# A fused Fourier transform and two expert layers on one core: three sequence passes and two means move in among the first items of the first tile

## The reference

```python
def _attn_ref(x):                        # x (2, 3008, 256)
    X = np.fft.fft(x, axis=1)
    X = np.fft.fft(X, axis=2)
    return X.real
def _moe_ref(x, w_gate, w_val, w_out, rms_g):      # d_ff 1536
    rms = np.sqrt(np.mean(x * x, axis=-1, keepdims=True) + 1e-06)
    xn = x / rms * rms_g
    g = xn @ w_gate
    silu = g * (1.0 / (1.0 + np.exp(-g)))
    return (silu * (xn @ w_val)) @ w_out
def _moe2_ref(x, w_in, w_out):                     # d_ff 2048
    h = x @ w_in
    return (h * np.cos(h)) @ w_out
```

## Time and profile before

| | |
|---|---|
| median of three runs | 978.87 us |
| the profiled execution's own time | 978.91 us |
| its span in the trace | 977.0 us |
| PE busy | 971.1 us (99%) |
| DVE, ACT, POOL busy | 742.1, 638.3, 350.6 us |
| granted PE clock | 0.999 |

### The profile page before, as it was taken

One profiled execution on the slowest core, in us unless ns is written; L12 is line 12 of the kernel. 1 busy time (PEld: TensorE's weight loads), 2 busy tenths in 40 slices (PEclk: granted clock), 3 DMA queues, 4 the chain that ended last, 5 costly groups with the idle time before them and its releaser, 6 DMA issues.

```text
span 977.0 us, 13033 instructions
## 1 busy us (share of the span) xinstructions
PE 971.1 (99%) x4530; PEld 808.7 (83%) x4530; DVE 742.1 (76%) x1029; ACT 638.3 (65%) x806; POOL 350.6 (36%) x291
## 2 busy tenths in 40 slices
PE   9999999999999999999999999999999999999998
PEld 8988888888888888888888888888888888888886
DVE  7888987678876768876768877767887667887665
ACT  5687787764378765368775358775348776447777
POOL 0477783047720027740007750006661004770000
PEclk9999999999999999999999999999999999999999
DMA  9888010001010001010001000001010000000001
GB/s 356 232 223 218 1 39 16 1 2 41 1 42 1 1 1 42 1 42 0 0 0 42 0 32 11 0 0 42 0 32 0 0 0 20 22 0 0 0 0 42
DMA packets 13794, 36.80 MB, mean 38 GB/s; under 512 B 2586, under 2 KB 6522, under 8 KB 13370
## 3 DMA queue, kind: packets, MB, share of 16 engines
q1 hardware_dynamic: 11690, 31.63, 9.3%
q0 software_dynamic: 2064, 4.72, 2.6%
HBM read 22.35 MB, written 9.26 MB: 32 GB/s over the span
## 4 chain that ended last, share of the span: by engine, by line
PE 98%; DVE 1%; DMA 0%; ACT 0%; issue 0%; DVEq 0%
PE ps L554 31%; PE ps L555 31%; PE ps L556 31%; PE ps L500 2%; PE ps L518 1%; PE ps L484 1%; PE ps L516 1%; DMA front<-x 0%; DVE plus L1028 0%; PE ps L540 0%; ACT g_sb L683 0%; DVE work L1036 0%; PE ps L481 0%; PE ps L480 0%; DVE work L1037 0%
## 5 line engine op out<-in xcount | busy, mean ns | idle before, releaser
L556 PE MATMUL ps<-h_hi,wo_lo 128*128 128x502 f32 x672 | 261.5, 389 | 0.0
L554 PE MATMUL ps<-h_hi,wo_hi 128*128 128x502 f32 x672 | 261.4, 389 | 0.0
L555 PE MATMUL ps<-h_lo,wo_hi 128*128 128x502 f32 x672 | 261.0, 388 | 0.0
L1127 POOL TENSOR_TENSOR h_lo<-work,h_hi 128x502 fp32r<-128x502 f32 x92 | 102.2, 1119 | 373.8 <-ACT h_hi L807 370.2
L792 ACT ACTIVATE h_hi<-work 128x502 fp32r<-128x502 f32 x132 | 82.2, 626 | 172.0 <-POOL work L1216 172.0
L1114 DVE SCALAR_TENSOR_TENSOR work<-work,ps 128x1004 f32<-128x1004 f32 (+1 forms) x109 | 117.2, 1075 | 95.3 <-ACT work L893 94.6
L1100 DVE SCALAR_TENSOR_TENSOR work<-work,ps 128x1004 f32<-128x1004 f32 (+1 forms) x109 | 116.5, 1074 | 48.4 <-ACT work L879 48.4
L554 PE MATMUL ps<-x_hi,win_hi 128*128 128x502 f32 x384 | 150.0, 391 | 0.0
L555 PE MATMUL ps<-x_lo,win_hi 128*128 128x502 f32 x384 | 149.4, 389 | 0.0
L556 PE MATMUL ps<-x_hi,win_lo 128*128 128x502 f32 x384 | 149.1, 388 | 0.0
L554 PEld LDWEIGHTS ps<-h_hi,wo_hi 128*128 128x128 f32 x672 | 126.2, 188 | 26.8 <-DVE h_lo L1021 0.6
(11 more groups left out here) (92 smaller groups left out, 1271.8 us busy)
## 6 DMA issues: line engine op xcount, KB each, us to landing
out<-y_sb SPq DMA_DIRECT2D x10, 502.0 KB, 3.2
front<-x SPq DMA_DIRECT2D x4, 768.0 KB, 9.0
w_lo<-w_f POOLq DMA_DIRECT2D x6, 512.0 KB, 7.0
uv_t<-uv_dram SPq DMA_DIRECT2D x6, 502.0 KB, 3.6
front<-x SPq DMA_DIRECT2D x4, 512.0 KB, 9.0
wo_raw<-wo SPq DMA_DIRECT2D x1, 2048.0 KB, 9.3
win_raw<-win SPq DMA_DIRECT2D x1, 2048.0 KB, 10.4
raw_b<-w1b SPq DMA_DIRECT2D x3, 512.0 KB, 12.6
```

The source lines that it names most:

```text
L554: nc.tensor.matmul(acc, w_hi, v_hi, start=start, stop=False)
L555: nc.tensor.matmul(acc, w_hi, v_lo, start=False, stop=False)
L556: return nc.tensor.matmul(acc, w_lo, v_hi, start=False, stop=stop)
L1127: nc.gpsimd.tensor_tensor(dst, src, hi.bitcast(F32), ALU.subtract).then_inc(s, 1)
```

## The change

What the edits do:

- `sequence(31)` is taken from before the first item and put into item 1; `sequence(32)` and `(33)` each move one place later. `rms(6)`, done at step 33 before, is done together with `rms(7)` inside item (2, 1), between the sum and the difference, in banks 6 and 7.
- On ACT, `uv_copy(15)` goes from before the first Silu to behind it; `mean_copy(6)` and `(7)` come behind `hi1(0)`.
- `pq` becomes four buffers, three of them behind `uv0` and one 2 KB behind `plus[0]`, so that `plus[0]` has bytes of its own.
- Two more weight slots, `w1_late0` and `w1_late1`, lie in the part of `wo1_hi` and `wo1_lo` that chunk 2 of wo1 fills later. Mixings no longer wait for `w1_lo_done`; chunks 4 and 5 are split on ACT in items 0 and 1 instead of 1 and 2; `split_wo1(2)`, in item 4, now waits for `w1_lo_done[4]` and `[5]`.
- Scalings and mixings are at other steps (the last two mixings at 25 and 33, not 31 and 32), and three small DVE instructions on the scale vectors come behind the copies of the transform's last groups.

```diff
@@
+        w1_late = [sb(f"w1_late{i}", [2, 512], o + 8192) for i, o in enumerate((o_o1h, o_o1l))]
+        def w1_slot(n):
+            return w1_f[:, n, :, :] if n < SLOTS else w1_late[n - SLOTS][:, :, :]
@@
-        pq = sb("pq", [4, DIM], o_pq)
+        pq = [sb(f"pq{i}", [DIM], o_h + UVB + 1024 * i if i < 3 else o_pq + 2048) for i in range(4)]
@@
-        RMS_AT = [8, 9, 15, 20, 24, 28, 33]
-        MEAN_COPY_AT = [2, 3, 7, 9, 11, 13, 14]
+        RMS_AT = [8, 9, 15, 20, 24, 28]
+        MEAN_COPY_AT = [2, 3, 7, 9, 11, 13]
@@
-            return 3 if q < len(RMS_AT) else 6 if q < MEANS - 1 else bank_pair(1)
+            return 3 if q < len(RMS_AT) else q if q < MEANS - 1 else bank_pair(1)
@@
-        MIX_AT = [3, 5, 8, 9, 16, 18, 20, 22, 24, 25, 31, 32]
+        MIX_AT = [3, 5, 7, 9, 11, 16, 18, 20, 22, 24, 25, 33]
...
-        W1_SPLIT_LATE, WO1_SPLIT_LATE = {1: 4, 2: 5}, {3: 1, 4: 2}
+        W1_SPLIT_LATE, WO1_SPLIT_LATE = {0: 4, 1: 5}, {3: 1, 4: 2}
@@ PE
-                if q == RMS_LATE[0]:
+                if q in RMS_LATE[:2]:
                     pe.wait_ge(uv_main, LAST - 2)
@@
-            sequence(LAST - 3)
@@
                 if first:
                     up1_sum(t, 1, 0)
-                    sequence(LAST - 2)
+                    sequence(LAST - 3)
                     up1_dif(t, 1, 0)
                     up1_sum(t, 1, 1)
-                    sequence(LAST - 1)
+                    sequence(LAST - 2)
                     up1_dif(t, 1, 1)
                     up1_sum(t, 2, 0)
-                    rms(RMS_LATE[0])
+                    sequence(LAST - 1)
                     up1_dif(t, 2, 0)
@@
-                    up1(t, i, halves=(1,))
+                    up1_sum(t, i, 1)
+                    if first and i == 2:
+                        rms(RMS_LATE[0])
+                        rms(RMS_LATE[1])
+                    up1_dif(t, i, 1)
@@ ACT
+                if n == WO1_CHUNKS - 1:
+                    act.wait_ge(w1_lo_done[SLOTS], 16)
+                    act.wait_ge(w1_lo_done[SLOTS + 1], 16)
@@
-            for p in range(LAST // 2 - 1):
+            for p in range(LAST // 2 - 2):
...
+            split_step(LAST // 2 - 2)
@@
+                    if first and i == 1:
+                        mean_copy(RMS_LATE[0])
+                        mean_copy(RMS_LATE[1])
                     act.wait_ge(g_ready, C1 * t + i + 1)
...
                     if first and i == 0:
+                        uv_copy(LAST // 2 - 2)
                         uv_copy(LAST // 2 - 1)
-                        mean_copy(RMS_LATE[0])
...
                     if first and i in W1_SPLIT_LATE:
                         split_w1(W1_SPLIT_LATE[i])
@@ DVE
-                if k // 2 >= SLOTS:
-                    dve.wait_ge(w1_lo_done[k // 2 - SLOTS], 16)
```

More of the change, by code:

```diff
@@ L111, in build @@
         wo1_raw = sb("wo1_raw", [C1 * DIM], o_i2h)
+        w1_late = [sb(f"w1_late{i}", [2, 512], o + 8192) for i, o in enumerate((o_o1h, o_o1l))]
+        assert WO1B == 3 * 4096 and 2 * FF1 == (SLOTS + 2) * 512
+        def w1_slot(n):
+            return w1_f[:, n, :, :] if n < SLOTS else w1_late[n - SLOTS][:, :, :]
         win2_hi, win2_lo = sb("win2_hi", [2 * FF2], o_i2h, F32R), sb("win2_lo", [2 * FF2], o_i2l, F32R)
@@ L154, in build @@
         o_pq = o_h + 4 * TA
-        pq = sb("pq", [4, DIM], o_pq)
+        pq = [sb(f"pq{i}", [DIM], o_h + UVB + 1024 * i if i < 3 else o_pq + 2048) for i in range(4)]
+        assert UVB + 3 * 1024 <= 4 * TA and 4 * N <= 2048
         zeros = sb("zeros", [P], o_pq)
@@ L237, in part_end, with parts_ending @@
             return b * STEPS + k.stop - 1
-        RMS_AT = [8, 9, 15, 20, 24, 28, 33]
-        MEAN_COPY_AT = [2, 3, 7, 9, 11, 13, 14]
+        def parts_ending(p):
+            return [q for q in range(MEANS) if part_end(q) // 2 == p]
+        RMS_AT = [8, 9, 15, 20, 24, 28]
+        MEAN_COPY_AT = [2, 3, 7, 9, 11, 13]
         RMS_LATE = range(len(RMS_AT), MEANS)
@@ L243, in build @@
         RECIP_LATE = {7: 1, 9: 2}
-        assert len(RMS_LATE) == 2
+        assert len(RMS_LATE) == 3 and not parts_ending(LAST // 2 - 2)
         def rms_bank(q):
-            return 3 if q < len(RMS_AT) else 6 if q < MEANS - 1 else bank_pair(1)
+            return 3 if q < len(RMS_AT) else q if q < MEANS - 1 else bank_pair(1)
         def rounds(q):
@@ L256, in quarters @@
             return min(4, PART_ROWS[q][1].stop - PART_ROWS[q][1].start) * QUARTER
-        def parts_ending(p):
-            return [q for q in range(MEANS) if part_end(q) // 2 == p]
         def means_copied(p):
@@ L515, in sequence @@
                 bank = 4 + G % 4
-                nc.tensor.matmul(ps[:, bank, 0:N2], pq[0:2 * H, slot(G), 0:P],
+                nc.tensor.matmul(ps[:, bank, 0:N2], pq[slot(G)][0:2 * H, 0:P],
                                  seq2[0:2 * H, k1, :], start=True, stop=True)
-                nc.tensor.matmul(ps[:, bank, N2:2 * N2], pq[0:2 * H, slot(G), P:DIM],
+                nc.tensor.matmul(ps[:, bank, N2:2 * N2], pq[slot(G)][0:2 * H, P:DIM],
                                  seq2[0:2 * H, k1, :], start=True, stop=True).then_inc(uv_done, 1)
@@ L650, in tile @@
                     if first and i == LAST_MEAN_AT:
-                        rms(RMS_LATE[1])
+                        rms(RMS_LATE[2])
                 down(t, C1 - 2)
@@ L741, in split_w1 @@
                 act.wait_ge(mixed, 2 * n + 2)
-                nc.scalar.activation(w1_hi[:, :, c], w1_f[:, n % SLOTS, :, :], ACT.Copy).then_inc(w1_hi_done, 1)
+                nc.scalar.activation(w1_hi[:, :, c], w1_slot(n), ACT.Copy).then_inc(w1_hi_done, 1)
                 if n >= W1_EARLY:
@@ L838, in tile @@
                     if first and i == LAST_MEAN_AT:
-                        mean_copy(RMS_LATE[1])
+                        mean_copy(RMS_LATE[2])
                     if first and i in W1_SPLIT_LATE:
@@ L1135, in w1_add @@
                     pool.wait_ge(w1_neg_late, n - W1_EARLY + 1)
-                pool.dma_start(w1_lo[:, :, c], w1_f[:, n % SLOTS, :, :], accum_op=ALU.add
+                pool.dma_start(w1_lo[:, :, c], w1_slot(n), accum_op=ALU.add
                                ).then_inc(w1_lo_done[n], 16)
```

18 lines of the change are left out of this document (9 added, 9 removed).

## The result

The changed kernel takes 980.47 us (median of 20 runs, 980.10 to 985.43), the kernel before 979.04 us (20 runs, 978.70 to 980.71). The forecast was 979.9 us. The profiled execution took 980.46 us with a span of 978.7 us, at a granted clock of 1.00, so it stands for the median, and the two spans differ by 1.7 us.

The account below looks back on a forecast made before the run. PE was taken to bound the first tile, with 0.7 us margin on the ACT chain before `down(0)`. Terms -0.12 + 0.88 + 0.3 gave +1.06 on 978.91: 979.97, median 979.9; 8-in-10 range 978.2 to 981.9.

Parts of the forecast that it names:

- The sum: Whole kernel: -0.12 + 0.88 + 0.3 = +1.06 us on the profiled 978.91, giving 979.97, or 979.9 for the median.
- the forecast's own range: Whole kernel: 979.2 to 980.8 us, for a late first `down` plus 0 to 0.9 of DMA waits; chance 0.56.
- main term: At `down(0)`: PE starts at 67.0 instead of 66.14, held by ACT's longer chain through `hi1(0)`; +0.88 us.
- Reading: First tile after 65.30: PE idles 0.06 us of 64.40, so earlier changes return one for one unless a new wait opens.
- Part 1: End of the transform: three small DVE instructions leave the place before the copy; between 0 and -0.28 us, taken as -0.12.
- Part 2: First item: its `pq` is no longer behind a mixing, so PE starts at 54.77, 0.87 us sooner.
- Part 3: PE before `down(0)`: with `sequence(31)` and `rms(6)` moved in, it could start at 65.7, 0.45 us sooner.
- Part 4: ACT before `hi1(0)`: uv copies and a split delay it to 65.2, `down(0)` to 67.0, +0.88; `down(1)` costs nothing.
- Part 5: DMA landings around `down(4)`: chunk 5 between 80.8 and 86.3, wo1's chunk 1 possibly late; 0.3 us for both.
- Rival A: At `down(0)`: ACT's new chain ends before PE needs it, so the gain arrives; -0.6, 978.3 us; chance 0.14.
- Rival B: At `down(4)`: ACT or PE waits for a DMA landing in full queues; up to 2.2 more, 981.8 us; chance 0.23.
- The rule of the Trainium skill: At `down(4)`: queues take turns, so an accumulating DMA beside one load takes about twice its time; no stall past the forecast.

Follow-up runs that it names:

- e1: Changed kernel with chunks 4 and 5 of the first weights split in items 1 and 2, not 0 and 1; 980.88 us, ratio 1.0019.
- e9: Changed kernel with the three small DVE instructions back in front of the transform's last copies; 980.63 us, ratio 1.0017.
- e2: Changed kernel with ACT's eight splits of the second input weights in items 7 to 10 instead of 6 to 9; 980.11 us, ratio 1.0016.
- f1: Changed kernel with the earlier kernel's weights' schedule (four slots, splits in items 1 and 2, no new wait), last two mixings at 29 and 33; 981.07 us, 1.0019.
- f2: f1 with ACT's splits of the second input weights in items 7 to 10 instead of 6 to 9; 979.53 us, ratio 1.0004.
- g2: f1 with the eleventh mixing at step 28 and chunk 5's scaling at step 23; 980.80 us, ratio 1.0017.
- g1: f2 with the eleventh mixing at step 28 and chunk 5's scaling at step 23; 979.55 us, ratio 1.0005.
- h1: Changed kernel, six slots, w1 splits in items 1 and 2, `split_wo1(2)` in item 5, second input weights' splits in items 7 to 10; 978.38 us, 0.9991.
- e3: Changed kernel with SP's 2 MB load of wo2 and the uv stores ahead of the spreading of means 6 and 7; 982.56 us, ratio 1.0043.
- e5: Kernel before with only the weights' part: two more slots, new steps, splits in items 0 and 1, the new wait; 980.56 us, ratio 1.0027.
- f3: Kernel before with ACT's eight splits of the second input weights in items 7 to 10 instead of 6 to 9; 979.75 us, ratio 1.0004.

## Why the prediction was right, and where it was not

The sum was +1.06 us; the profiled execution shows +1.7, the medians +1.43. The time is inside the forecast's own range, and its main term was right in place and size, but that term was not the one that set the end: a second bound moved by 1.72 us, more than the whole sum. For waits on DMA the prediction had 0.3 on top of the main term, and they made 0.75. From the traces the sum is -0.11 + 0.98 + 0.75 = +1.62.

- **Reading.** "Comes back at the end one for one, unless a new wait opens later": the condition failed. From the earlier trace rows, 0.06 us idle, I took the stage for bound by PE alone. A bound that stands at PE's pace shows next to no idle time either, and this one did (two starts of 0.34 and 0.33 us at `down(11)`): with nothing gained in front of it nothing is seen, and what is gained is swallowed (e1). Behind the second layer it does hold, 849.3 us in every kernel.
- **Part 1**, -0.12: right. The first features at 23.19 against 23.20 look like 0.01, but the fold ended 0.10 later in that trace; counted from the fold it is 0.11, and e9 takes it back.
- **Part 2**, first item at 54.77: 54.82. DVE's first `plus_part` at 56.48: 56.52.
- **Part 3**, PE able to start `down(0)` at 65.7: in e1, where nothing holds it, it starts at 65.55, 42.19 from the first features, 0.75 sooner than before and not 0.45. What moved costs 0.3 to 0.4 less than added up. So PE idles 1.55 us in front of the first `down` and not 1.2.
- **Part 4**: copy at 62.8 (62.77), split at 63.2 (63.15), `hi1(0)` at 65.2 (65.20), `down(0)` at 67.0 (67.10). +0.88 forecast, +0.96 measured, and +0.98 at layer 2 where nothing else stands (e2). That `down(1)` costs nothing held too: no wait there in the changed kernel. "From item 2 on ACT has no split and catches up" is the step that failed: ACT has splits in items 3, 4 and 6 as well, and those of items 4 and 6 stand behind DMA landings.
- **Part 5**, the load at 67.6 (67.59) and chunk 5's landing between 80.8 and 86.3 (71.88 + 12.5 = 84.4) held, and so did no stall at `down(4)`: by 1 us for the new wait, and by 0.6 for chunk 1 of wo_lo, which landed at 89.1 for a `down(4)` at 89.72. The term of 0.3 is the mis-sized one, and its place was wrong: 0.75 (after against e2) was lost at `down(10)` and `down(11)`. I had costed the nearest landings and not the last of the line. ACT stood in the new wait until 84.43, so chunk 2 of wo_lo was issued at 88.19 instead of 84.63, landed at 96.7 instead of 94.9, and ACT's item 6 came 1.72 later. The kernel before showed this wait of ACT, 4.41 us at 95.05, and it is easily read as idle time of an engine with slack. DVE's remainder of item 6, 26.88 us in front of layer 2 in both kernels, waits for that ACT row:

```profile
98.98 1.15 DVE L1028 TENSOR_TENSOR h_lo<-work,h_hi 128x502 fp32r<-128x502 f32 x1 [0.44 <-ACT h_hi L806]
```

The pairs after/e2 (0.75), f1/f2 (1.3) and g2/g1 (1.0) show it by taking that one wait, and the two splits behind it, out of item 6.

- **Rival A** was wrong for the change as made, and right for what the moved passes can bring: h1 has it. **Rival B** did not happen in the changed kernel, and did in e1 (1.2) and e3 (2.1): it stood 0.6 us away, so a chance of 0.23 was not too high.
- **The rule of the Trainium skill**, "DMA: Bandwidth & Descriptors", section on queues, rings and completion order, has queues take turns; by that an accumulating DMA beside one load takes twice its time alone. The shortest landing of this size here is 4.6 us (e5, chunk 0 of wo_lo), and twice that is 9.2. Chunk 2 of wo_lo beside the load of the second input weights took 7.7 to 11.5 us, on both sides of it, so one landing priced by the rule can be 2 us off. Chunks 4 and 5 of the changed kernel took 12.0 and 12.5; they had a load, the stores of uv and each other beside them, so they are no test of it, and the measurement decides. No stall past the forecast at `down(4)` came true all the same.

What stays open is what makes one landing of the same DMA 3 us longer than another in the same program (f1 and f2); no run took the other transfers away one by one.

## What to carry to other kernels

An engine's long wait for a DMA is not slack when the engine behind it then runs without a pause to the end of the stage, and a full PE doesn't exclude such a bound (0.06 us idle here): follow the released instruction to the next place where PE could wait, and count parallel bounds by the later one, not by their sum. Work that is moved to use a free place delays everything behind it on the same in-order engine, here a queue of DMAs that each release the next; check every later landing, not the nearest. A load put ahead can cost more than it brings: look at what starts sooner because of it, here the next load, and at what is then in flight. Before two traces are compared by their times, count both from an instruction that the change doesn't touch, and as near as possible: a front that ran 0.10 us later hid the whole of part 1.

## What the runs showed of the hardware

Accumulating DMAs of one size (512 KB) from SBUF to SBUF, chunks of w_lo and wo_lo, took 4.6 to 12.6 us from issue to landing in the fourteen traces. Chunk 2 of wo_lo took 5.0 in h1, where the load beside it was ending (issued at 92.61, the load landed at 93.5); beside the 2 MB load of the second input weights it took 7.7 to 9.1 in ten traces and 10.1 to 11.5 in three (before, f3, f1). Chunks 4 and 5 of the changed kernel took 12.0 and 12.5 beside the load of wo2, the stores of uv and each other.

DVE and POOL slowed each other down when both worked from SBUF. In f2 the split of uv on DVE took 1.82 us beside POOL's scaling of 1.90 us; in the changed kernel, where they overlap by 0.1 us, 1.20 and 1.24. A mixing, 0.74 us alone, took 1.88 beside POOL's addition of squares (1.16, the last row below):

```profile
52.76 1.82 DVE L980 TENSOR_TENSOR uv_lo<-uv_t,uv_hi 128x1004 fp32r<-128x1004 f32 x1
54.50 1.26 DVE L970 SCALAR_TENSOR_TENSOR pq<-feat,ps 96x256 f32<-96x256 f32 x3
55.69 1.88 DVE L1001 SCALAR_TENSOR_TENSOR w_f<-raw_a,gvec,raw_b 128x512 f32<-128x512 f32 x1
```

```profile
51.61 1.90 POOL L1190 TENSOR_TENSOR u<-u,inv_t 128x502 f32<-128x502 f32 x1
53.52 1.76 POOL L1166 TENSOR_TENSOR squares<-squares 128x376 f32<-128x376 f32 x1
...
55.85 1.16 POOL L1166 TENSOR_TENSOR squares<-squares 128x376 f32<-128x376 f32 x1
```

The Trainium skill, "GPSIMD Engine Reference", section Specifications, says that POOL's SBUF access is shared with DVE, with contention for DVE instructions with two SBUF inputs; these rows agree. The mixing and the addition together took 1.88 us; in the changed kernel, where they overlap by 0.3 us, they took 0.74 and 1.00, so here the pair paid about the sum. A mixing at step 29 or 33 can cost more than its 0.74 us for this, and doesn't always: at step 33 it took 1.88 in f2 and 0.74 in the changed kernel.
